# Counting the ranks of the first chunk on VectorE instead of TensorE, in an attention, gated-product and routed-experts kernel

## The reference

```python
cap = N // E                      # 1536 // 8 = 192
logits = x @ w_gate               # [N, E]
order = np.argsort(-logits.flatten())
for idx in order:
    tok, e = idx // E, idx % E
    if assigned[tok] >= 0 or counts[e] >= cap:
        continue
    assigned[tok] = e
    counts[e] += 1
...
out[mask] = np.maximum(x[mask] @ w1[e], 0.0) @ w2[e]    # mask = assigned == e
```

## Time and profile before

| | before |
|---|---|
| median of 3 runs | 644.66 us (643.49 to 645.02) |
| profiled execution | 644.6 us, of it the span 642.9 us |
| PE busy | 627.3 us, 98% of the span |
| PEld busy | 520.7 us, 81% |
| DVE busy | 312.9 us, 49% |
| ACT busy | 258.2 us, 40% |
| POOL busy | 317.0 us, 49% |
| one-column matmuls of the counts (L1124) | 624, 23.0 us busy |
| granted clock of TensorE, mean | 0.997 |

### The profile page before, as it was taken

The page is one execution under the profiler, slowest core; times in us unless marked ns, Lnnn a source line. Parts: engine busy times, 40 slices in busy tenths (PEclk is TensorE's granted clock), DMA queues, the critical chain, the costliest instruction groups (busy, mean ns, idle before and its releaser), DMA issues.

```text
span 642.9 us, 13224 instructions
## 1 busy us (share of the span) xinstructions
PE 627.3 (98%) x4909; PEld 520.7 (81%) x4909; DVE 312.9 (49%) x1085; ACT 258.2 (40%) x639; POOL 317.0 (49%) x229
## 2 busy tenths in 40 slices
PE   8999999999999999999999999999789999999995
PEld 5666669989899899989977777777688889888894
DVE  5888882111134227725898997888611121112110
ACT  5898893233332332332332224222524442344330
POOL 7656563545455445445456551000087555865561
PEclk9999999999999999999999999999999999999998
DMA  8374232334454463445214151413469656875400
GB/s 275 100 274 149 77 92 67 99 104 124 148 161 122 130 188 109 130 116 183 68 34 148 51 180 34 149 50 126 155 232 361 235 198 219 301 271 195 167 25 24
DMA packets 76094, 94.35 MB, mean 147 GB/s; under 512 B 4448, under 2 KB 53888, under 8 KB 75392
## 3 DMA queue, kind: packets, MB, share of 16 engines
q1 hardware_dynamic: 73696, 86.82, 40.9%
q0 software_dynamic: 2048, 6.29, 3.2%
q10 hardware_dynamic: 288, 0.41, 0.2%
HBM read 87.16 MB, written 6.34 MB: 145 GB/s over the span
## 4 chain that ended last, share of the span: by engine, by line
PE 94%; DVE 2%; DMA 1%; issue 1%; POOL 0%; ACT 0%; POOLq 0%; DVEq 0%
PE bank L1230 15%; PE bank L1112 14%; PE bank L1326 13%; PE bank L1114 13%; PE bank L1113 13%; PE bank L1347 4%; PE bank L1038 4%; PE bank L1099 4%; PE bank L1058 4%; PE bank L1124 2%; PE bank L1273 1%; PE bank L1185 1%; PE bank L1104 1%; PE bank L1052 1%; PE bank L1311 1%; PE bank L1014 1%
## 5 line engine op out<-in xcount | busy, mean ns | idle before, releaser
L500 POOL TENSOR_TENSOR wl_ab<-raw_ab,wh_ab 128x1024 fp32r<-128x1024 f32 x46 | 110.1, 2393 | 117.0 <-ACT wh_ab L607 117.0
L1112 PE MATMUL bank<-xh,wh_ab 128*128 128x384 f32 x384 | 133.0, 346 | 0.0
L1114 PE MATMUL bank<-xh,wl_ab 128*128 128x384 f32 x384 | 128.7, 335 | 0.0
L1113 PE MATMUL bank<-xl,wh_ab 128*128 128x384 f32 x384 | 128.6, 335 | 0.0
L570 POOL TENSOR_TENSOR w2l<-w_raw,w2h 128x1024 fp32r<-128x1024 f32 x32 | 75.1, 2378 | 43.6 <-ACT w2h L721 43.5
L859 DVE TENSOR_TENSOR hid<-hid,bank 128x384 f32<-128x384 f32 x48 | 26.6, 554 | 127.0 <-ACT hid L621 127.0
L1326 PE MATMUL bank<-xgT,w_sb 128*128 128x192 f32 x512 | 86.4, 327 | 0.9 <-DVE xgT L986 0.9
L1326 PEld LDWEIGHTS bank<-xgT,w_sb 128*128 128x128 f32 x512 | 83.3, 190 | 2.0 <-issue 1.0
L621 ACT ACTIVATE hid<-bank 128x384 f32<-128x384 f32 x48 | 23.6, 492 | 150.1 <-PE bank L1114 150.1
L1112 PEld LDWEIGHTS bank<-xh,wh_ab 128*128 128x128 f32 x384 | 72.0, 188 | 8.9 <-issue 8.3
L837 DVE TENSOR_SCALAR_CACHE_REDUCE ge<-lb,L 128x384 bf16<-128x384 f32 (+2 forms) x72 | 72.8, 1011 | 3.3 <-PE bank L1124 3.3
(11 more groups left out here) (143 smaller groups left out, 1016.3 us busy)
## 6 DMA issues: line engine op xcount, KB each, us to landing
w_sb<-in_moe_w_dram SPq DMA_DIRECT2D x8, 2048.0 KB, 8.0
w_raw<-in_moe_w_dram SPq DMA_DIRECT2D x32, 512.0 KB, 6.6
raw_ab<-in_moe_w_a_dram SPq DMA_DIRECT2D x48, 256.0 KB, 2.9
raw_ab<-in_moe_w_b_dram SPq DMA_DIRECT2D x48, 256.0 KB, 3.3
raw_out<-in_moe_w_out_dram SPq DMA_DIRECT2D x24, 256.0 KB, 2.6
lb<-logit_rows SPq DMA_DIRECT2D x4, 1536.0 KB, 6.6
v_sb<-in_v_dram SPq DMA_DIRECT2D x8, 384.0 KB
woT<-in_moe_w_outT_dram SPq DMA_DIRECT2D x1, 3072.0 KB, 10.8
```

The lines of the kernel that those rows point to most:

```text
L500: pool.tensor_tensor(wl_ab[s % 2][:, :], raw_ab[s % 3][:, :], wh_ab[s % 2][:, :].bitcast(F32), ALU.subtract).then_inc(abl_done, 1)
L1112: pe.matmul(dst, lh, rh, start=first, stop=False)
L1113: pe.matmul(dst, lh, rl, start=False, stop=False)
L1114: return pe.matmul(dst, ll, rh, start=False, stop=last)
```

## The change

For chunk 0 (m < 24, tiles 0 to 2) VectorE makes a second compare for each group, with the tokens of the chunk from the own tile on: 384, 256 and 128 columns for t = 0, 1, 2. It asks whether the other token is at most as large (`is_le`) and multiplies with a second mask in PSUM, `LATER`, which is -1 for larger indices and 0 else; its sum goes into the free column 0 of `rank_parts`. The mask is written once, at step 9 of chunk 0, into columns 128 to 511 of bank LATE by two VectorE instructions. TensorE makes no counts for chunk 0; its counting begins with chunk 1 (steps of chunk 2). VectorE's wait before a compare is now, for chunk 0 and the first four groups after it, on its own compares of four groups earlier, and the counts awaited after that are 24 fewer.

```diff
--- before.py
+++ after.py
@@ -83,6 +83,10 @@
         return (t // TC * E + e) * TC + t % TC
 
 
+    def counts_before(m):
+
+        return max(0, m - E * TC)
+
     def rows_before(m):
 
         return max(0, m - E * TC)
@@ -292,7 +296,7 @@
         routed = sem("routed")
         parts_cleared, ge_ready, ge_diag, ge_counted = (sem("parts_cleared"), sem("ge_ready"), sem("ge_diag"),
                                                         sem("ge_counted"))
-        mask_up = sem("mask_up")
+        mask_up, later_up, ge_later = sem("mask_up"), sem("later_up"), sem("ge_later")
         atleast_ready, counted = sem("atleast_ready"), sem("counted")
         chosen_ready, pos_ready, names_ready, idx_counted, idx_ready = (
             sem("chosen_ready"), sem("pos_ready"), sem("names_ready"), sem("idx_counted"), sem("idx_ready"))
@@ -309,6 +313,7 @@
         SB_, PT_, OB_, TB = banks[0:3], banks[3:5], banks[5:7], banks[7]
 
         AB_, BB_, LT_, LG, LATE = banks[0:2], banks[2:4], banks[4:6], banks[6], banks[7]
+        LATER = LATE[:, P:P + C]
         OWN, WOG = LG[:, P:P + C], LG[:, 0:NF * E]
         YB_ = [banks[i] for i in (0, 2, 1, 3, 5, 4)]
         CNT, POS = banks[6], banks[6]
@@ -828,10 +833,13 @@
                 m = group_of(t, e)
                 g = ge[m % 4]
                 li = L[:, t, e:e + 1]
-                if m >= 4:
-
-                    dve.wait_ge(ge_counted, m - 3)
                 c, own = t // TC, P * (t % TC + 1)
+                if m >= 4 and m < E * TC + 4:
+                    dve.wait_ge(ge_later, m - 3)
+                    dve.wait_ge(ge_diag, m - 3)
+                if m >= E * TC + 4:
+
+                    dve.wait_ge(ge_counted, counts_before(m - 3))
                 if c > 0:
                     earlier = g[:, 0:C * c].rearrange("p (c t) -> p c t", c=c)
                     dve.tensor_scalar(earlier, lb[:, 0:c, e, :], li, 0.0, ALU.is_ge, ALU.add,
@@ -839,6 +847,11 @@
                 dve.scalar_tensor_tensor(out=g[:, C * c:C * c + own], in0=lb[:, c, e, 0:own], scalar=li,
                                          in1=OWN[:, C - own:C], op0=ALU.is_ge, op1=ALU.mult,
                                          accum_out=rank_parts[:, t, e, 1:2]).then_inc(ge_diag, 1)
+                if c == 0:
+                    later = C + P - own
+                    dve.scalar_tensor_tensor(out=g[:, C:C + later], in0=lb[:, 0, e, C - later:C], scalar=li,
+                                             in1=LATER[:, 0:later], op0=ALU.is_le, op1=ALU.mult,
+                                             accum_out=rank_parts[:, t, e, 0:1]).then_inc(ge_later, 1)
 
             def compare_of_step(s, k):
 
@@ -847,6 +860,7 @@
                     if c == 1 and f == F_COMPARE and k == 0:
                         dve.wait_ge(parts_cleared, 1)
                         dve.wait_ge(mask_up, 1)
+                        dve.wait_ge(later_up, 2)
                     if f == F_COMPARE and k == 0:
                         dve.wait_ge(lb_in[c - 1], 16)
                         dve.wait_ge(l_out, c)
@@ -871,6 +885,10 @@
                     wog_copy(GATE_AT.index(s - 2))
                 if s + 1 < STEPS:
                     compare_of_step(s, 2)
+                if s == GATE_AT[-1] + 2:
+                    dve.wait_ge(gateT_out, len(GATE_AT))
+                    dve.tensor_scalar(LATER[:, 0:P], before16[:, :], -1.0, None, ALU.mult).then_inc(later_up, 1)
+                    dve.memset(LATER[:, P:C], -1.0).then_inc(later_up, 1)
                 if s % NF == 2 and s > NF:
                     l_copy(s // NF - 1)
             compare_of_step(STEPS - 1, 0)
@@ -907,8 +925,9 @@
                     compare(t, e)
             dve.wait_ge(ge_ready, rows_before(GROUPS))
             dve.wait_ge(ge_diag, GROUPS)
+            dve.wait_ge(ge_later, E * TC)
             link(dve.tensor_reduce(parts[:, :, :], rank_parts[:, :, :, :], AX.X, ALU.add))
-            dve.wait_ge(ge_counted, GROUPS)
+            dve.wait_ge(ge_counted, counts_before(GROUPS))
             link(dve.tensor_tensor(upper[:, :, :], LATE[:, 0:NT * E].rearrange("p (t e) -> p t e", t=NT),
                                    base_rn[:, :, :], ALU.add))
 
@@ -1116,20 +1135,22 @@
             def count_group(t, e):
 
                 m = group_of(t, e)
+                if t == TC and e == 0:
+                    pe.wait_ge(later_up, 2)
                 if t >= TC:
                     pe.wait_ge(ge_ready, rows_before(m + 1))
                 pe.wait_ge(ge_diag, m + 1)
                 for j in range(t + 1):
 
                     mm = pe.matmul(LATE[:, j * E + e:j * E + e + 1], ge[m % 4][:, j * P:(j + 1) * P],
-                                   ones16[:, 0:1], start=(m == 0 and j == 0), stop=(m == GROUPS - 1 and j == t),
+                                   ones16[:, 0:1], start=(m == E * TC and j == 0), stop=(m == GROUPS - 1 and j == t),
                                    skip_group_check=True)
                 mm.then_inc(ge_counted, 1)
 
             def count_groups(s):
 
                 c, f = s // NF, s % NF
-                if c > 0 and F_COMPARE <= f < F_COMPARE + E:
+                if c > 1 and F_COMPARE <= f < F_COMPARE + E:
                     for t in range(TC * (c - 1), TC * c):
                         count_group(t, f - F_COMPARE)
```

## The result

The changed kernel takes 640.52 us (median of 10 runs, 639.17 to 641.34) against 644.84 of the kernel before (10 runs, 642.09 to 646.48). The ratio is 0.994, with a 95% interval of 0.9925 to 0.9955: 3.9 us faster (2.9 to 4.8; the medians lie 4.3 apart), where 1.9 was forecast. The profiled execution took 640.6 us, its span 638.9 against 642.9.

What follows compares the result with a forecast made beforehand. TensorE's queue was taken as the bound: 8 x 0.29 = 2.3 us saved, less three waits of 0.13, taken as 1.9, with nothing for added DVE work; 644.66 - 1.9 = 642.7 us, range 641.7 to 644.0.

Steps and rivals of the forecast that it cites:

- the bound (TensorE's queue): Whole kernel: TensorE is busy 98% of the span, so only shortening or holding up its queue moves the end.
- the price of a block: Chunk 1 steps: removing six one-column count matmuls saves 0.29 us of the beat, 2.3 us for eight blocks.
- what is given back: Bare steps of chunk 1: the chain over GpSimd makes beats 4.16 and 4.29 in turn; three waits of 0.13 us.
- the eighth step's full 0.29: Eighth step with counts: logit matmuls before the wide ones cover the chain, so it saves its full 0.29 us.
- the sum there: Steps of chunk 1: 1.67 us saved in seven steps plus 0.29 in the eighth, 1.96 us together.
- A: Chunk 1 steps: GpSimd's result comes in time, nothing is given back; 2.3 us saved, 642.3 us; chance 0.15.
- B: Chunk 1 steps: 4.29 in every step, 1.4 us saved, 643.2; or a block worth 0.26, 643.0; chance 0.17.
- C: Chunk 1 steps: DVE's new compares hold up GpSimd's L500; 3.1 us slower, 647.8 us; chance 0.05.
- D: Chunk 1 steps: something else held TensorE there, the beat stays 4.454; 644.7 us; chance 0.04.
- E: Chunk 1 steps: only each block's own 0.16 us is won; 0.9 us saved, 643.8 us; chance 0.04.
- step (d) of what is added: SyncE and GpSimd queues, DMA: nothing moves or changes, and the lead is carried to the end.
- The prediction's own sign: Eighth step's end to span's end should stay 418.1 us; otherwise the step carrying the lead to the end is wrong.

Runs made afterwards that it cites:

- e3_compare_and_count: Changed kernel with TensorE's counts of chunk 0 kept beside the new compares, into a bank nobody reads; ratio 0.9984 to the kernel before.
- e6_after_padded: Changed kernel with 96 TensorE instructions more at its very start, so its program is as long as before; ratio 0.9986 to the kernel before.
- e2_after_again: Changed kernel run again without any edit; 640.11 us, ratio 0.9949 to the kernel before.
- e11_after_third: Changed kernel, unedited, third trace; 118.60 us from first product copy to the eighth step's end, 1.26 us from routing's end to gather.
- e7_before_padded: Kernel before with 160 TensorE instructions more at its start, so fetches fall as in the changed kernel; ratio 1.0003 to the kernel before.
- e1_before_again: Kernel before run again without any edit; 644.34 us, ratio 1.0002.
- e10_before_fourth: Kernel before, unedited, fourth trace; 120.51 us from first product copy to the eighth step's end, 3.59 us from routing's end to gather.
- e4_no_count_no_compare: Changed kernel without its second compares, so neither counts nor compares for the later tokens of chunk 0; ratio 0.9947 to the kernel before.
- e8_compare_thrice: Changed kernel with each second compare on VectorE made three times; 644.25 us, one execution.

## Why the prediction was wrong, step by step

**Right, to a tenth:** the bound (TensorE's queue); the price of a block, 0.29 us; what is given back, 4.17 and 4.30 in turn, with three steps longer by about 0.13, of which two showed a wait for GpSimd (0.16 us each); the eighth step's full 0.29; the sum there, 1.96 worked out and 1.90 measured. The compares on DVE cost nothing, the mask writes took 0.28 and 0.27 (the bound was 0.555 each), L859 stayed 0.53 behind L621. Rivals A and B fall by the beat, C by e3_compare_and_count and the even 2.40 us of L500, D and E by the beat. E's sum had an error of its own: with 0.16 us won a step the beat is 4.454 - 0.16 = 4.29, over the 4.225 of the chain, so nothing is given back, and E stood for 1.3 us and not for 0.9.

**Wrong:** step (d) of what is added, "Nothing moves on the SyncE and GpSimd queues, and no DMA changes", and with it that the lead is carried to the end unchanged. The prediction's own sign for it came: from the eighth step's end to the span's end it is 638.9 - 221.78 = 417.1 us, not 418.1. One kind of DMA did change, the fetches of TensorE's program. The page lists them (q8 instruction, 40 packets, 0.66 MB); the prediction has no term for them. 96 instructions less moved one fetch out of the last store of y, which is on the path: the gather, GpSimd and TensorE wait for it. That is worth 2.3 us in the traces, more than the change itself. The DMA wait was visible before, too: the last store landed in 4.4 us where the median of its kind is 2.5, in the view of y_rows:

```profile
DMA to landing us min/median/max: 2.0/2.5/4.4
```

The sum by stretches is 1.9 + 2.3 = 4.2 us. The two measured ratios give 3.9 us (2.9 to 4.8) and 3.3 us (2.1 to 4.5), the medians of the same sets 4.3 and 3.9, so both hold it. Nothing is to be taken off for the fall of the clock, as it is as frequent before. Nor does it follow TensorE's shorter wait before the experts: it fell in e6_after_padded with the long wait, and not in e2_after_again, e11_after_third and e7_before_padded with the short one.

It was luck, for both kernels, where a fetch stood against the last store. The second half of the gain is real and repeats, but it belongs to this program's length and not to the idea of the change.

The range was too narrow for a second reason: it was built from the terms of the steps alone, with nothing for a stretch that I had declared untouched.

## What to carry to other kernels

An edit that changes the number of an engine's instructions shifts all later fetches of its program, and a fetch of 0.9 to 1.9 us can hold up a transfer that other work waits for (here by 1.8 to 2.5 us). Look for stores or loads on the path that land late in the trace (here 4.4 us against 2.5), and see in the DMA view whether an instruction packet lies in them. In the changed kernel one store of y still lands in 4.1 us, and nothing waits for it: what counts is the one on the path. Such luck can be moved by adding or taking away instructions anywhere ahead. Where an engine sets the beat, price what is taken off it from the beat of the steps and not from busy time, and then look which chain had been just as long: here it took back 0.4 of 2.3 us, and turning two ScalarE operations round returned it, and as much again from steps elsewhere.

## What the runs showed of the hardware

- A 16 KB instruction packet took 0.9 to 1.9 us. Where one of 1.6 to 1.9 us fell into the last store of y (before, e1_before_again, e10_before_fourth, e3_compare_and_count, e6_after_padded), the store's last packets came about 2 us behind the rest, and the gather waited 3.6 to 3.7 us instead of 1.25.
- A six-matmul block of one column cost 0.29 us of the beat with 164 ns of busy time a matmul; removing all eight by themselves (e4_no_count_no_compare) and with 24 DVE compares in their place gave the same beat.
- DVE could run some 4 us late against TensorE, summed over the steps, before TensorE waited (an estimate from e8_compare_thrice).
- The mean granted clock of a whole execution was 0.996 or less in 33 of 60 executions of the kernel before and in 9 of 18 of the changed one.
